# Local attention with global keys first in each 128-key set, overlapping value reads, one load of global parts a batch, and late expert weights

## The chip, the cores and the metric

The kernel runs on one core of a Trainium2 chip. The metric is the device time of one execution in microseconds (us), lower is better.

## What is computed

Three parts follow one another: local attention with global tokens, a mixture of four attention experts, and a channel mixing. Only the first and the weights of the second matter here (B = 4 batches, H = 8 heads, Sl = 512 local and Sg = 32 global tokens, head width 64, all float32):

```python
k_all = np.concatenate([k_g, k_l], axis=2)
v_all = np.concatenate([v_g, v_l], axis=2)
s_g = scale * np.matmul(q_g, k_all.transpose(0, 1, 3, 2))
out_g = np.matmul(sm(s_g), v_all)                      # sm: softmax
s_ll = scale * np.matmul(q_l, k_l.transpose(0, 1, 3, 2))
mask = np.abs(pos[:, None] - pos[None, :]) <= 32
s_ll = np.where(mask, s_ll, -1000000000.0)
s_lg = scale * np.matmul(q_l, k_g.transpose(0, 1, 3, 2))
a_l = sm(np.concatenate([s_lg, s_ll], axis=-1))
out_l = np.matmul(a_l, np.concatenate([v_g, v_l], axis=2))
```

The experts then use `moe_wq`, `moe_wk`, `moe_wv` (4 x 512 x 64 each), `moe_wo` (4 x 64 x 512) and `moe_w_gate` (512 x 4).

## The kernel before

**Tiling.** Each string of 32 local queries sees 32 global keys and at most 96 local ones, so its keys are a set of 128, and the keys' 128 rows are one contraction when the values are weighed. Four heads are a half of a batch (hf 0 and 1), two heads a pair. A *unit* u is half of the queries of a pair: 8 strings for each of 2 heads, 16 small matmuls of 32 rows of scores by 128 keys. A half has six steps: four units of local queries (v = 0 to 3), one of all global queries against all keys (v = 4), and one (v = 5) without scores of its own, in which the second part of the global result is turned and weighed. A batch has 12 steps (`UB`), and the four batches run through one software pipeline.

**Order.** Each engine has its own hand-written queue, and the engines meet at semaphores. At step i TensorE turns the probabilities of unit i-3 (`turn_probs`), perhaps keys, queries or global parts of what comes (tables `K_AT`, `Q_AT`, `G_AT`), turns back the result of unit i-6 (`turn_back`, tile `ps_X`), weighs values with unit i-4 (`weigh`, `ps_O`) and forms the scores of unit i (`scores`, `ps_S`). VectorE adds the mask and takes maxima (`maxima`), ScalarE takes exponentials and evicts (`exps`, `keep_probs`, `keep_out`). The global parts of the next batch's first half are turned at step 9; the first weighing of a half is at its steps 4 or 10.

**Keys.** The keys of a pair lie in `KS` as one string of 22 blocks of 32, in which a copy of the global keys stands every 128 columns, so each window of 128 columns holds the 32 global keys at some place (`window`). VectorE writes the local blocks (L592, L594), GpSimd the copies of the global ones (`keys_global`, L330).

**Values.** `VW` holds 14 windows of 128 rows in the same orders. `load_v` (L256) loads windows 0 to 4 and one quarter of window 9 in 11 transfers, and `copy_v` (L267) makes the others from them within SBUF by 6 more, which wait for all 11. `load_v` of batch b may start for a half when that half of batch b-1 has been weighed to its end (the semaphore `weighed`); for the second half this is step 3 of the following batch.

**The queue of SP.** All of these transfers are issued by SP, in order: for each batch queries, keys and global parts of both halves (`load_qk`), then loads and copies of values of the first half, then of the second. In batch 0 the 15 transfers of expert weights (L284 to L293) follow.

**Splitting of weights.** Each weight is split into a high part (ScalarE, L572) and a low one (GpSimd, L337), in 16 pieces at steps 6 to 11 of batch 0. The first split waits for all 15 transfers. The first use of the weights is behind the last batch, in `expert_projection`.

## Time and profile before

| what | value |
|---|---|
| median of 3 runs | 652.73 us (652.26 to 654.95) |
| the profiled execution | 655.85 us |
| span in the profile | 654.1 us |
| mean granted TensorE clock | 0.955 |
| busy: TensorE matmul, VectorE, ScalarE, GpSimd | 578.7, 321.4, 276.8, 96.3 us |
| attention stage | 0 to 186 us |
| its transfers | 36.2 MB in 75409 packets over the whole span, most of them of 256 bytes |

The waits show, for each engine, who made it idle; the timeline gives each group of instructions with its start; the windows give the busy time of each engine, the granted clock and the rate of the DMA engines for a stretch. A matmul in float32 leaves two records in the trace (x32 for 16 matmuls); a transpose leaves one. A row of the timeline gives start, duration of the whole group, engine, line, operation, and in brackets how long the engine had been idle and for whom.

### The profile page before, as it was taken

How to read it: one execution, taken by the hardware profiler on the slowest of the kernel's cores; microseconds unless marked ns; L12 is line 12 of the kernel's file. 1: busy time of each engine (PE TensorE's matmuls, PEld its weight loads, DVE VectorE, ACT ScalarE, POOL GpSimd, SP SyncE). 2: the span in 40 equal slices, each digit the busy share in tenths (PEclk: the TensorE clock that was granted, in tenths of full speed). 3: DMA queues.
4: the chain of work that ended last, by engine and by line, in shares of the span. 5: the costliest groups of instructions: out<-in, count | busy, mean ns of one | idle time of the engine just before them, and what ended most of it. 6: DMA issues, size and time to landing. Idle time of an engine off the chain costs nothing. (4 is left out here: it accounts for less than half of the span.)

```text
span 654.1 us, 16023 instructions
## 1 busy us (share of the span) xinstructions
PE 578.7 (88%) x6100; PEld 478.2 (73%) x6100; DVE 321.4 (49%) x807; ACT 276.8 (42%) x733; POOL 96.3 (15%) x189
## 2 busy tenths in 40 slices
PE   5718976896898899989989979799999999999998
PEld 3516654674685598779759749688989899898986
DVE  5424756575625435634653684754435344343412
ACT  3409756585645534533544453534133141322301
POOL 2006100010036412221232331300000000000000
PEclk9976989798999699989999998999999999999999
DMA  6697576766022100000000000400000000000000
GB/s 150 153 214 159 116 166 159 172 153 156 3 67 80 33 2 2 2 1 0 0 1 17 2 1 2 130 33 1 32 16 16 32 0 32 0 32 16 17 33 16
DMA packets 75409, 36.23 MB, mean 55 GB/s; under 512 B 68320, under 2 KB 68320, under 8 KB 75360
## 3 DMA queue, kind: packets, MB, share of 16 engines
q1 hardware_dynamic: 75360, 35.56, 22.0%
q8 instruction: 33, 0.54, 0.4%
q14 instruction: 16, 0.13, 0.1%
HBM read 21.77 MB, written 4.46 MB: 40 GB/s over the span
## 5 line engine op out<-in xcount | busy, mean ns | idle before, releaser
L44 PE MATMUL ps_H<-XH,w_kL 128*128 128x256 f32 (+1 forms) x288 | 81.5, 283 | 1.2 <-ACT square L1514 1.2
L1514 ACT ACTIVATE square<-ps_H 128x512 f32<-128x512 f32 (+1 forms) x36 | 20.5, 573 | 143.7 <-PE ps_H L46 141.6
L46 PE MATMUL ps_H<-XH,w_kH 128*128 128x256 f32 (+1 forms) x288 | 81.0, 281 | 0.0
L45 PE MATMUL ps_H<-XL,w_kH 128*128 128x256 f32 (+1 forms) x288 | 81.0, 281 | 0.0
L44 PEld LDWEIGHTS ps_H<-XH,w_kL 128*128 128x128 f32 x288 | 54.8, 190 | 2.1 <-ACT square L1514 1.4
L44 PE MATMUL ps_V<-w_vH,HL 128*128 128x512 f32 x136 | 53.8, 396 | 2.1 <-DVE HL L1566 2.1
L45 PEld LDWEIGHTS ps_H<-XL,w_kH 128*128 128x128 f32 x288 | 54.9, 190 | 0.4
L46 PEld LDWEIGHTS ps_H<-XH,w_kH 128*128 128x128 f32 x288 | 54.8, 190 | 0.0
L45 PE MATMUL ps_V<-w_vL,HH 128*128 128x512 f32 x136 | 53.7, 395 | 0.0
L46 PE MATMUL ps_V<-w_vH,HH 128*128 128x512 f32 x136 | 53.5, 394 | 0.0
L1582 DVE TENSOR_TENSOR square<-square 128x512 f32<-128x512 f32 (+1 forms) x36 | 24.4, 680 | 45.3 <-ACT square L1514 45.3
L1067 ACT ACTIVATE probs_m<-ps_H,nmax_m 128x128 f32<-128x128 f32 (+3 forms) x64 | 33.2, 523 | 31.0 <-DVE nmax_m L1221 30.9
L1599 DVE TENSOR_TENSOR gate<-ps_V,gate 128x512 f32<-128x512 f32 x17 | 11.8, 692 | 64.5 <-PE ps_V L46 64.5
L530 ACT ACTIVATE probs<-probs,nmax 128x128 f32<-128x128 f32 x128 | 40.7, 392 | 4.9 <-DVE nmax L623 4.9
L619 DVE TENSOR_TENSOR probs<-ps_S,mask 128x512 f32<-128x512 f32 x32 | 22.1, 691 | 40.9 <-PE ps_S L410 40.8
L538 ACT ACTIVATE PTs<-ps_P 128x512 f32<-128x512 f32 (+1 forms) x48 | 26.8, 559 | 34.5 <-PE ps_P L426 34.2
L1342 POOL TENSOR_SCALAR probs_m<-probs_m,rinv_m,coef 128x128 f32<-128x128 f32 (+3 forms) x64 | 39.2, 622 | 0.0
L449 PE MATMUL ps_O<-VW,PTs 128*32 128x65 f32 x1024 | 22.7, 233 | 15.8 <-DMA VW<-VW 14.9
L462 PE MATMUL ps_X<-ident,xn 128*128 128x128 f32 x72 | 15.8, 294 | 22.8 <-ACT xT L553 19.0
L449 PEld LDWEIGHTS ps_O<-VW,PTs 128*32 128x32 f32 x1024 | 17.5, 116 | 22.2 <-issue 20.7
L1221 DVE TENSOR_REDUCE nmax_m<-ps_H 128x1 f32<-128x128 f32 (+3 forms) x64 | 28.4, 484 | 10.9 <-PE ps_H L921 10.7
L44 PEld LDWEIGHTS ps_V<-w_vH,HL 128*128 128x128 f32 x136 | 25.9, 190 | 8.2 <-DVE HL L1566 2.6
(238 smaller groups left out, 1435.9 us busy)
## 6 DMA issues: line engine op xcount, KB each, us to landing
out_dram<-gate SPq DMA_DIRECT2D x17, 256.0 KB, 2.0
QKn<-in_k_l_dram SPq DMA_DIRECT2D x32, 128.0 KB, 2.6
QKn<-in_q_l_dram SPq DMA_DIRECT2D x32, 128.0 KB, 2.8
VW<-in_v_l_dram SPq DMA_DIRECT2D x40, 96.0 KB, 2.1
VW<-VW SPq DMA_DIRECT2D x24, 130.0 KB, 3.7
VW<-VW SPq DMA_DIRECT2D x8, 325.0 KB, 3.6
VW<-VW SPq DMA_DIRECT2D x8, 260.0 KB, 3.9
raw_b<-in_moe_w_k_dram SPq DMA_DIRECT2D x8, 256.0 KB, 2.8
```

The source lines that it names most:

```text
L44: nc.tensor.matmul(out, al, bh, start=(starts and k == 0), stop=False)
L45: nc.tensor.matmul(out, ah, bl, start=False, stop=False)
L46: last = nc.tensor.matmul(out, ah, bh, start=False, stop=(ends and k == n - 1))
L449: last = nc.tensor.matmul(out[SG * k:SG * k + SG, at:at + VD], PTs[:, u % 2, 2 * r + n, SG * k:SG * k + SG], VW[:, hf, w, 2 * (pair % 2) + ...
L530: last = nc.scalar.activation(pr, pr, ACT.Exp, bias=nmax[:, place(u), at:at + 1])
L538: nc.scalar.activation(PTs[:, u % 2, 0:n, :].rearrange("p j q -> p (j q)"), ps_P[:, u % 2, 0:P * n], ACT.Copy).then_inc(pt_kept, 1)
L619: nc.vector.tensor_tensor(pr, ps_S[:, :, 0:2 * P].rearrange("p r (n k) -> p r n k", n=2), mask[:, 2 * t:2 * t + 2, :, :].rearrange("p n a ...
L1067: nc.scalar.activation(probs[:, slot, r, 0:n], ps_S[:, r, 0:n], ACT.Exp, bias=nmax[:, slot, r:r + 1], accum_out=den[:, slot, r:r + 1]).the ...
L1221: nc.vector.tensor_reduce(nmax[:, slot, r:r + 1], ps_S[:, r, 0:n], AX.X, ALU.max, negate=True).then_inc(maxed, 1)
L1342: last = nc.gpsimd.tensor_scalar(pr, pr, rinv[:, slot, r:r + 1], coef[:, i, 2 * ep + r:2 * ep + r + 1], ALU.mult, ALU.mult)
L1514: nc.scalar.activation(square[:, g % 2, 0:2 * n], ps_H[:, g % 2, 0:2 * n], ACT.Relu).then_inc(relued, 1)
L1582: nc.vector.tensor_tensor(square[:, g % 2, 0:2 * n], square[:, g % 2, 0:2 * n], square[:, g % 2, 0:2 * n], ALU.mult).then_inc(squared, 1)
```

## The change

- The keys lie in `KS` as they come, 512 columns, evicted by one copy. The global keys stay in `GT`. Each set of 128 keys is now 32 global ones first, then 96 local ones, and its scores come from two matmuls: 96 columns from `KS`, 32 from `GT`. GpSimd's copies and the semaphore `kg_kept` go. The masks are the same in all strings but the first and the last.
- The values' window w is the 96 local rows from 32w on; all 14 are read from memory by one transfer per head (rows are read up to three times). The global rows are loaded once into window 0 and copied to the other 13 by one transfer.
- Global queries and keys come by two transfers a batch instead of four, behind the queries and keys of the first half.
- The expert weights come by 5 transfers instead of 15, issued behind the values of batch 1, and are split in 17 pieces at steps 2 to 10 of batch 3.
- A first exponential on ScalarE stands ahead of the first eviction.

```diff
@@ attention_phase @@
     def window(s):
-        c, kind = divmod(min(max(s, 1), 14) - 1, 3)
-        return 4 * c + (0, 2, 3)[kind], (0, 5, 10)[kind] + c
+        return min(max(s, 1), NW) - 1
...
-        SPLIT_FROM = 6
+        SPLIT_FROM = 2
...
         def split_at(b, i):
-            if isinstance(b, int) and b == 0 and i >= SPLIT_FROM:
+            if isinstance(b, int) and b == B - 1 and SPLIT_FROM <= i < UB:
...
+                def load_g(b):
+                    if b:
+                        sp.wait_ge(g_turned, 2 * b)
+                    for kind, glo in enumerate((qg_h, kg_h)):
+                        sp.dma_start(Gn[:, kind, :, :], glo[H * b:H * b + H, :, :].rearrange("h p d -> p h d")).then_inc(g_loaded, 16)
...
                 def load_v(b, hf):
-                    for c in range(5):
-                        sp.dma_start(VW[0:SG, hf, c, :, 0:DH], vg_h[h, :, :].rearrange("h p d -> p h d")).then_inc(v_loaded[hf], 16)
-                        sp.dma_start(VW[SG:P, hf, c, :, 0:DH],
-                                     vl_h[h, 96 * c:96 * c + 96, :].rearrange("h p d -> p h d")).then_inc(v_loaded[hf], 16)
-                    sp.dma_start(VW[96:P, hf, 9, :, 0:DH],
-                                 vl_h[h, SL - SG:SL, :].rearrange("h p d -> p h d")).then_inc(v_loaded[hf], 16)
+                    sp.dma_start(VW[0:SG, hf, 0, :, 0:DH], vg_h[h:h + 4, :, :].rearrange("h p d -> p h d")).then_inc(vg_loaded[hf], 16)
+                    for n in range(4):
+                        v = vl_h[h + n, 0:P - SG, :]
+                        sp.dma_start(VW[SG:P, hf, :, n, 0:DH],
+                                     bass.AP(v.tensor, v.offset, [[DH, P - SG], [SG * DH, NW], [1, DH]])).then_inc(v_loaded[hf], 16)
-                def copy_v(b, hf):
+                def copy_vg(b, hf):
                     sp.wait_ge(pool_set, POOL_SET)
-                    sp.wait_ge(v_loaded[hf], 16 * V_LOADS * (b + 1))
...
+                    sp.wait_ge(vg_loaded[hf], 16 * (b + 1))
+                    sp.dma_start(VW[0:SG, hf, 1:NW, :, :].rearrange("p w h d -> p w (h d)"),
+                                 VW[0:SG, hf, 0, :, :].rearrange("p h d -> p (h d)").unsqueeze(1)
+                                 .to_broadcast([SG, NW - 1, 4 * VD])).then_inc(vg_copied[hf], 16)
...
-                with sp.Fori(1, B) as b:
+                for b in range(1, B):
                     load_qk(b, 0)
+                    load_g(b)
                     load_qk(b, 1)
                     load_v(b, 0)
-                    copy_v(b, 0)
+                    copy_vg(b, 0)
                     load_v(b, 1)
-                    copy_v(b, 1)
+                    copy_vg(b, 1)
+                    if b == 1:
...
@@ scores @@
                     for n in range(2):
-                        for k in range(4):
...
-                                last = nc.tensor.matmul(ps_S[SG * k:SG * k + SG, r, P * n:P * n + P],
-                                                        QT[rows, pair % 2, SG * s:SG * s + SG], KS[rows, pair, at:at + P],
-                                                        start=True, stop=True)
+                        for local in (True, False):
+                            for k in range(4):
...
+                                    if local:
+                                        nc.tensor.matmul(out[:, SG:P], q, KS[rows, pair, at:at + P - SG], start=True, stop=True)
+                                    else:
+                                        last = nc.tensor.matmul(out[:, 0:SG], q, GT[rows, hf, pair % 2, :], start=True, stop=True)
...
@@ ScalarE, ahead of its first eviction @@
+                act.wait_ge(dve_set, 1)
+                nc.scalar.activation(nmax_g[:, 0:1], zerob[:, 0:1], ACT.Exp)
@@ keep_keys @@
-                    nc.vector.tensor_copy(KS[:, pair, 0:5 * P].rearrange("p (c k) -> p c k", k=P)[:, :, SG:P],
-                                          ps_T[:, 0:480].rearrange("p (c k) -> p c k", c=5))
-                    nc.vector.tensor_copy(KS[:, pair, 5 * P + SG:STRING], ps_T[:, 480:SL]).then_inc(k_kept, 1)
+                    nc.vector.tensor_copy(KS[:, pair, :], ps_T[:, :]).then_inc(k_kept, 1)
```

On TensorE, in batch 0 about its steps 6 and 7, the rows before are these (a name left of the arrow is the tile written, right of it the tiles read; sizes are partitions by columns):

```order
L449 MATMUL ps_O<-VW,PTs 32x65 x16
L410 MATMUL ps_S<-KS,QT 32x128 x16
L426 MATMUL ps_P<-ident,probs_g 128x128 x4
L376 MATMUL ps_T<-ident,QKn 128x128 x4
L462 MATMUL ps_X<-ident,xn 128x128 x2
```

and now:

```order
L438 MATMUL ps_O<-VW,PTs 32x65 x16
L398 MATMUL ps_S<-KS,QT 32x96 x8
L400 MATMUL ps_S<-GT,QT 32x32 x8
L398 MATMUL ps_S<-KS,QT 32x96 x8
L400 MATMUL ps_S<-GT,QT 32x32 x8
L414 MATMUL ps_P<-ident,probs_g 128x128 x4
L361 MATMUL ps_T<-ident,QKn 128x128 x4
L451 MATMUL ps_X<-ident,xn 128x128 x2
```

The 16 score matmuls of a unit have become 32, in four groups of 8; the rest stands where it stood.

On SP, before, the end of batch 0 with the second half's copies and the expert weights (the loop over batches 1 to 3 begins behind them):

```order
L264 DMA VW<-in_v_l_dram 32x4x64
L273 DMA VW<-VW 64x1300
L273 DMA VW<-VW 32x1300
L273 DMA VW<-VW 32x1040 x3
L273 DMA VW<-VW 64x1040
L284 DMA raw_qk<-in_moe_wq_dram 128x4x64 x4
L284 DMA raw_qk<-in_moe_wk_dram 128x4x64 x4
L287 DMA raw_v<-in_moe_wv_dram 128x4x64 x4
L289 DMA raw_v<-in_moe_w_gate_dram 128x4x4
L292 DMA raw_o<-in_moe_wo_dram 128x512 x2
```

and now, from the values of the second half of batch 1 to the global parts of batch 2:

```order
L264 DMA VW<-in_v_g_dram 32x4x64
L268 DMA VW<-in_v_l_dram 96x14x64 x4
L275 DMA VW<-VW 32x13x260
L296 DMA raw_qkv<-in_moe_wq_dram 128x16x64
L296 DMA raw_qkv<-in_moe_wk_dram 128x16x64
L296 DMA raw_qkv<-in_moe_wv_dram 128x16x64
L298 DMA raw_g<-in_moe_w_gate_dram 128x4x4
L299 DMA raw_o<-in_moe_wo_dram 128x2x512
L256 DMA QKn<-in_k_l_dram 128x4x64 x2
L256 DMA QKn<-in_q_l_dram 128x4x64 x2
L256 DMA QKn<-in_k_l_dram 128x4x64 x2
L256 DMA QKn<-in_q_l_dram 128x4x64 x2
```

The weights have moved a batch back, and the two transfers of `Gn` for batch 2 (L247) come right behind this piece.

## Rows read from the trace of the kernel before

**Rows 1.** Waits to 190 us: who waited for whom, us in total, times, longest.

```profile
ACT WQH L572 <- DMA raw_o<-in_moe_wo_dram: 15.4, 1, 15.4
PE ps_O L449 <- DMA VW<-VW: 14.9, 3, 5.4
...
PE ps_T L353 <- DMA Gn<-in_k_g_dram: 6.5, 2, 3.3
```

**Rows 2.** Timeline of TensorE: the first global-query matmuls of the eight halves.

```profile
26.62 1.87 PE L398 MATMUL ps_S<-KS,GQ 128*64 128x480 f32 x4
...
60.24 1.03 PE L398 MATMUL ps_S<-KS,GQ 128*64 128x480 f32 x4
...
75.75 1.03 PE L398 MATMUL ps_S<-KS,GQ 128*64 128x480 f32 x4
...
95.69 1.03 PE L398 MATMUL ps_S<-KS,GQ 128*64 128x480 f32 x4
...
116.64 1.87 PE L398 MATMUL ps_S<-KS,GQ 128*64 128x480 f32 x4
...
133.35 1.03 PE L398 MATMUL ps_S<-KS,GQ 128*64 128x480 f32 x4
...
153.33 1.87 PE L398 MATMUL ps_S<-KS,GQ 128*64 128x480 f32 x4
...
169.07 1.03 PE L398 MATMUL ps_S<-KS,GQ 128*64 128x480 f32 x4
```

**Rows 3.** Timeline of TensorE and SP's queue around the waits in batches 0 and 1.

```profile
51.23 0.66 PE L462 MATMUL ps_X<-ident,xn 128*128 128x128 f32 x2 [15.45 <-ACT xT L553]
...
69.71 0.41 PE L462 MATMUL ps_X<-ident,xn 128*128 128x128 f32 x2 [0.56 <-ACT xT L553]
...
72.91 0.43 PE L440 MATMUL ps_O<-VW,PTs 128*32 128x65 f32 x16
...
82.22 4.63 SPq L273 DMA_DIRECT2D VW<-VW  x6
87.66 0.32 SPq L247 DMA_DIRECT2D Gn<-in_q_g_dram  x1
...
90.27 0.19 PE L353 MATMUL ps_T<-zerob,identb 128*128 128x32 bf16 x1 [3.24 <-DMA Gn<-in_k_g_dram]
```

**Rows 4.** Timeline rows of small matmuls, and their own rows (ns min/median/max).

```profile
15.04 1.11 PE L410 MATMUL ps_S<-KS,QT 64*32 64x128 f32 x32 [0.85 <-DVE probs L619]
...
83.73 0.67 PE L410 MATMUL ps_S<-KS,QT 64*32 64x128 f32 x32
...
274.62 0.66 PE L954 MATMUL ps_Mm<-PTs_m,VS 128*64 128x32 f32 x16 [0.50 <-DVE PTs_m L1152]
...
L410 PE MATMUL ps_S<-KS,QT x1024: 269/269/420, 11.0 to 167.4; 64*32 64x128 f32 x171
...
L954 PE MATMUL ps_Mm<-PTs_m,VS x128: 214/223/315, 219.7 to 383.4; 128*64 128x32 f32 x128
```

**Rows 5.** Timeline of the start: ScalarE's table load, TensorE's first weighing.

```profile
4.14 1.28 ACT L503 ACT_TABLE_LOAD   x1 [4.14 <-PE ps_T L357]
...
25.59 1.10 PE L449 MATMUL ps_O<-VW,PTs 128*32 128x65 f32 x32 [4.76 <-DMA VW<-VW]
```

**Rows 6.** Windows: us, busy of PE, PEld, DVE, ACT, POOL; PEclk, DMA share, GB/s.

```profile
31.00:36.00 5.00, 4.78 (x147) 3.56 (x145) 4.15 (x12) 1.27 (x4) 0.00 (x0) 1.00 0.77 184
...
42.00:46.00 4.00, 0.00 (x0) 0.00 (x0) 0.00 (x0) 0.00 (x0) 0.00 (x0) 0.50 1.09 215
...
101.00:108.00 7.00, 6.33 (x200) 4.80 (x188) 5.08 (x14) 4.84 (x17) 0.00 (x0) 1.00 0.61 138
...
125.00:130.00 5.00, 4.37 (x144) 3.14 (x143) 4.00 (x11) 4.33 (x13) 0.00 (x0) 1.00 0.87 195
```

**Rows 7.** ScalarE's splits in the timeline, and a window of batch 3 (columns as above).

```profile
47.66 1.03 ACT L572 ACTIVATE WQH<-raw_qk 128x256 fp32r<-128x256 f32 x3 [15.39 <-DMA raw_o<-in_moe_wo_dram]
...
160.00:166.00 6.00, 5.30 (x170) 3.74 (x153) 5.37 (x13) 4.92 (x15) 0.00 (x0) 1.00 0.30 69
```

More of the change, by code:

```diff
@@ L276, in _ @@
+                load_g(0)
                 load_qk(0, 0)
@@ L337, in split_weights @@
                     nc.gpsimd.tensor_tensor(lo, src, hi, ALU.subtract).then_inc(w_split, 1)
-                def step(b, i):
-                    turn_at(b, i, K_AT, keys_global)
-                    for n in split_at(b, i):
-                        split_weights(n)
-                turn_at(0, -1, K_AT, keys_global)
-                run(pool, step, 0)
+                for n in range(len(pieces)):
+                    split_weights(n)
             @block.tensor
```

140 lines of the change are left out of this document (58 added, 82 removed).

## The prediction

> **What bounds the kernel now.** I read first the page, then the waits of the first 190 us, then the timeline of TensorE, last the DMA share by stage. TensorE is the busiest engine, but the change touches only the attention stage, the first 186 us; the code behind it is the same, so all terms lie in front. There the waits [rows 1] name three losses: 15.4 us in one piece, in which ScalarE waits for the last expert weight and holds up all that is queued behind it, TensorE's transpose at 51.23 among it [rows 3]; 14.9 us in three pieces in which the first weighing of a batch waits for the copied value windows; and 6.5 us for the global queries and keys (3.24 of it at 90.27).
>
> As a ruler I take the first global-query matmul (L398) of each half batch [rows 2]: 26.62, 60.24, 75.75, 95.69, 116.64, 133.35, 153.33, 169.07. The eight stand six steps apart. The one clean distance is 60.24 to 75.75, **15.5 us**. Seven of these would be 109 us; the rows show 142. What is over is the waits and the slow clock behind them: 51.23 to 60.24 took 9.0 us at a granted clock of 0.50 (the level of 1.2 GHz), while the same piece at full clock, 69.71 to 75.75, took 6.0 [rows 2, 3, 6]. So a long wait costs its length and about 3 us more, a wait of 5 us about 1.3 more (116.64 to 133.35 is 16.7).
>
> What feeds those waits is the SP queue. It works in order, 54 transfers a batch, and the copies of values can only be issued once the loads have landed: from the weighing that frees a half's values (ends 73.3) the values alone hold the queue until 86.9, and the next batch's loads start at 87.66 [rows 3]. From batch 2 to batch 3 the ruler shows 36.7 us against 31 for two clean halves.
>
> **The change part by part.**
>
> *Scores, more matmuls (cost).* Each of the 32 score groups goes from 16 matmuls to 32 (96 and 32 columns in place of 128). The trace shows two records for each such matmul, so 64 for 32. Two prices are possible. The group of 32 takes 0.67 us with a last record of 0.269: (0.67 - 0.269)/31 = 12.9 ns from one to the next [rows 4]. If the streamed columns set this, the total of columns stays and the cost is about nil. If the load of 32 stationary columns sets it, 32 more records cost 32 x 12.9 = 0.41 us. The nearest row with few streamed columns is L954: 32 of them behind 64 stationary ones, (0.66 - 0.214)/15 = 29.7 ns apart [rows 4]. By streamed columns it should be quicker than L410; it is twice as slow, and has twice the stationary columns. So I take **0.41 us per group**, with 0.03 and 0.60 (a whole group again) as ends. Global queries: 480+64 columns become 512+32, nothing. Per half four groups, 1.64 us. Of this one group fills the gap of half a us in which TensorE now waits for ScalarE (0.56 at 69.71) [rows 3], and a clean half becomes 15.5 + 1.64 - 0.4 = **16.8 us**.
>
> The Trainium skill, TensorEngine Tiling (Array Packing), section Performance Considerations, says against this that a matmul costs some 60 cycles however few columns it has. On eight tiles side by side 32 more records would then cost 32 x 60 / 8 cycles, 0.1 us by an estimate from that page, and the sum would be some 6 us better.
>
> *Values by overlapping reads.* Per half 17 transfers become 6. The bytes hardly move: 0.69 MB loaded and 1.16 MB copied before; 1.41 MB loaded and 0.43 MB copied now. But the copy needs only the small global load, so no landing stands in the queue, and the 4.63 us in which SP issues six copies [rows 3] become one issue. The DMA engines become the limit. Their rate when nothing holds them is 215 GB/s, at a share over 1; 184 at 0.77 with copies; 195 at 0.87; 138 at 0.61 where SP's small issues limit [rows 6]. I take 212 GB/s for all, and 195 and 224 as ends. Per half: values 8.7 us, queries and keys (1.05 MB) 4.9 us, together 13.6, less than 16.8. So the waits for values in front of 116.64 and 153.33, 5 us each, go.
>
> On this the Trainium skill, DMA: Bandwidth & Descriptors, section Specifications, has a rule: below 512 bytes a transfer does not reach line rate. Here 256-byte rows ran at 195 GB/s for a share of 0.87 and mostly 4 to 5 KB rows at 184 for 0.77, 224 against 239 per full share; were 256 bytes to run at half of the copies' rate, the sum would turn to a loss (third rival).
>
> *Start (A).* The table load (1.28 us) leaves the path [rows 5]; larger global loads give some back, -0.9. Four score groups at the low clock cost 4 x 0.68 (0.41 x 1.11/0.67), less the 0.85 us gap at 15.04 [rows 4]. TensorE came to the first weighing at 25.59 - 4.76 = 20.8 [rows 5], now 20.8 - 0.9 + 1.9 = 21.8. The values need 4.07 MB through the DMA engines: 0.8 + 0.4 + 19.2 + 2.6 = 23.0. L398 about 1.1 later, 24.1: **-2.5**.
>
> *Weights late.* In batch 0 the 15.4 us wait and its slow clock go. But the same 2.1 MB now stand in the SP queue behind the values of batch 1's second half and **ahead of batch 2's queries, keys and global parts**. SP may issue those values only once the last weighing of batch 0 is done (step 3 of batch 1). In the trace: weighing ends at 73.3, global load issued at 87.66, in use at 90.27, where TensorE had waited 3.24 [rows 3]. Now, counted from that weighing: values 1.84 MB, weights 2.11, queries and keys 1.05, at 212 GB/s 23.6 us, and 2.7 for issue, transfer and landing of the global parts (87.66 to 90.27): 26.3. TensorE wants them at step 9, 87.0 - 73.3 = 13.7 us after the weighing before, now some 15.0 (four score groups more, less the gap). **Wait of about 11.4 us in batch 1.** Without weights (batch 2) it is 13.6 + 2.7 = 16.3 against 15.0: 1.3. In batch 0: 6.96 MB from the start, 0.8 + 0.4 + 32.8 + 2.6 = 36.6, against L398 + 12.1 = 36.2 for TensorE: 0.4.
>
> *One load of global parts.* Same bytes, 2 issues fewer; but it now stands behind the queries and keys instead of ahead of them, 4.9 us later. Counted above; it is what makes the two small waits.
>
> *ScalarE in batch 3.* 17 splits of some 0.31 us (1.03 us for three) move from batch 0, where they ran beside stalled work, to steps 2 to 10 of batch 3. ScalarE is busy 4.92 of 6.00 us there [rows 7], 2.1 of a step of 2.6. Two splits add 0.6 and the longer step, 2.8, leaves 0.7: it just fits, so each late piece now reaches TensorE. From 0 to 4 us (the 4.9 that the splits take, less what is free); I take 1.0. *VectorE, GpSimd:* the key eviction is one copy instead of two, the 16 fills by GpSimd go, the masks are 14 small writes instead of 32 and end before the first sum: nothing on the path, as TensorE does not wait for them.
>
> **The sum**, half by half (now minus before): A -2.5; B 33.6 to 16.8 + 0.4 + 0.7 of slow clock (half of 1.3), -15.7; C 15.5 to 16.8, +1.3; D: the weighing that frees the values ends 2.4 + 0.4 before L398, the wait 26.3 after it (23.5 after L398), then 4.3 + 0.4 + 2.8 of slow clock to the next L398, 31.0 for 19.9, +11.1; E 16.8 + 0.7 for 20.95, -3.4; F 16.8 + 1.3 for 16.7, +1.4; G 16.8 for 19.98, -3.2; H 16.8 + 1.0 for 15.7, +2.1. Together **-8.9 us**. The profiled execution took 655.85 us (span 654.1), 3 us above the median; I put the difference on the median: 652.73 - 8.9 = **643.8 us**.
>
> **The rivals.**
> 1. *Score matmuls cost nothing* (columns bound them). C, E, G, H lose 1.2 each, B and F some 0.8, since there the DMA engines set the time: -15.3, 637.4 us. Against it L954. The Trainium skill leans this way with the 60 cycles of its page TensorEngine Tiling (Array Packing), section Performance Considerations.
> 2. *The DMA engines give 195 GB/s*, as in the mixed stage. B +2.9, D +2.0, F +1.2, and waits of 2.6 us at step 9 of batches 0 and 2 now bring the low clock, as the 3.24 us one did, 1.3 each: about 652.7 us, no change. The gain is given back as waits for global parts.
> 3. *The value reads are slow* (**slower than before**). They are 5376 packets of 256 bytes per half for 2688, in steps of 8 KB in memory. Each extra us per half lands on A, B, D and F and brings slow clock of 3 to 4 us in all: the sum turns when a half's reads take some 1.5 to 2 us more than 6.5, below 165 GB/s. At 140 GB/s they take 9.8: +13 and +4, 661 us. For it: nothing in the rows, all loads are of 256 bytes already. Against: 215 GB/s for expert weights, most of them in 256-byte rows.
> 4. *ScalarE sets batch 3*: its end of 4 us instead of 1, and one spell of slow clock, 1.3: 648.1 us.
>
> **How the numbers follow.** Forecast 0.45 (640 to 648), rival 1 0.16, rival 2 0.15, rival 3 0.13, rival 4 0.11. The range takes in 1, 2 and 4 and leaves 3 out: 635 to 656 us. A measurement of this kernel tells about 0.5% from no change, 3.3 us. Faster than 649.5: forecast, rival 1 and most of 4, 0.70; within: rival 2 and the rest, 0.16; slower 0.14.
>
> **What would show it.** The score group's two rows together: 1.08 us or 0.70. TensorE's wait for Gn at step 9 of batch 1, about 11 us, under 2 in batches 0 and 2; none for VW after the first. Clean halves of 16.8 us; the DMA rate over 200 GB/s while values load; the last L398 near 160. A wait for VW in later batches, or a wait for Gn over 3 us in batch 2, would show the value reads slower than I took them. If the prediction is wrong by much, the likely step is the wait behind the weights, the largest term that is only worked out.

## The result and the profile after

The changed kernel takes **661.32 us** (median of 9 runs, 658.63 to 663.21) against 652.73 (9 runs): ratio 1.0125, interval 1.0103 to 1.0148. It is slower by 8.6 us where 8.9 us less were forecast, and the time lies outside the range of 635 to 656. The profiled run has a span of 661.0 us. Attention ends at 193.0 us instead of 186, so nearly all of the difference stands where the forecast put all of its terms. Executions more than 1.5% above the fastest of their kernel are left out of every median and ratio in this document (one of four of a_wide_gap_gfirst, three of eleven of a_gap_gfirst and three of ten of a_unroll, among the experiments below).

TensorE's rows after the change: six of the eight ruler matmuls (L382 now, to be laid beside [rows 2]) and every stop of over 1 us between 5 and 150 us.

```profile
24.92 1.09 PE L438 MATMUL ps_O<-VW,PTs 128*32 128x65 f32 x32 [4.16 <-DMA VW<-VW]
25.95 1.98 PE L382 MATMUL ps_S<-KS,GQ 128*64 128x512 f32 x4
...
42.09 0.19 PE L338 MATMUL ps_T<-zerob,identb 128*128 128x32 bf16 x1 [3.05 <-DMA Gn<-in_k_g_dram]
...
47.53 1.08 PE L382 MATMUL ps_S<-KS,GQ 128*64 128x512 f32 x4
...
64.67 1.08 PE L382 MATMUL ps_S<-KS,GQ 128*64 128x512 f32 x4
...
77.73 1.08 PE L429 MATMUL ps_O<-VW,PTs 128*32 128x65 f32 x29 [2.39 <-issue]
...
89.41 0.20 PE L338 MATMUL ps_T<-zerob,identb 128*128 128x32 bf16 x1 [9.37 <-DMA Gn<-in_k_g_dram]
...
95.33 1.08 PE L382 MATMUL ps_S<-KS,GQ 128*64 128x512 f32 x4
...
104.63 1.11 PE L414 MATMUL ps_P<-ident,probs 128*128 128x128 f32 x4 [6.41 <-issue]
...
119.49 1.08 PE L382 MATMUL ps_S<-KS,GQ 128*64 128x512 f32 x4
...
135.51 0.21 PE L338 MATMUL ps_T<-zerob,identb 128*128 128x32 bf16 x1 [2.62 <-DMA Gn<-in_k_g_dram]
...
142.20 1.08 PE L382 MATMUL ps_S<-KS,GQ 128*64 128x512 f32 x4
```

The last two L382 stand at 159.38 and 176.06. Piece by piece (A is the time up to the first of them, B to H are the distances from one to the next):

| | A | B | C | D | E | F | G | H | last L382 |
|---|---|---|---|---|---|---|---|---|---|
| forecast | 24.1 | 17.9 | 16.8 | 31.0 | 17.5 | 18.1 | 16.8 | 17.8 | 160.0 |
| measured | 25.95 | 21.6 | 17.1 | 30.7 | 24.2 | 22.7 | 17.2 | 16.7 | 176.06 |
| miss | +1.9 | +3.7 | +0.3 | -0.3 | +6.7 | +4.6 | +0.4 | -1.1 | +16.1 |

The clean halves (C, G) and the piece with the big wait behind the weights (D) came out near the forecast. Three pieces carry most of the miss. B and F end in waits for `Gn`, as the forecast had them, but of 3.05 and 2.62 us for 0.4 and 1.3. And in E stands something that it didn't have at all: at 104.63 TensorE had been idle for 6.41 us, "issue", that is, for nothing that the profile shows. No such row is in the kernel before. L414 there is the first work of a pass of TensorE's loop over batches 1 and 2: the stop is at the jump back to the loop's start.

Two views tell more. First the page's DMA queues (packets, MB, share of the 16 engines). Of the kernel before:

```profile
q1 hardware_dynamic: 75360, 35.56, 22.0%
q8 instruction: 33, 0.54, 0.4%
...
HBM read 21.77 MB, written 4.46 MB: 40 GB/s over the span
```

Of the changed kernel:

```profile
q1 hardware_dynamic: 97472, 35.47, 25.8%
q8 instruction: 49, 0.80, 0.6%
...
HBM read 27.54 MB, written 4.46 MB: 48 GB/s over the span
```

The data queue moves the same bytes in 29% more packets. And q8, an instruction queue with packets of 16 KB, has 49 packets instead of 33; the runs below show that it follows the length of TensorE's code. Between 100 and 140 us, the loop's second pass, the kernel before fetches none and the changed one nine. The DMA view of these 40 us of the changed kernel:

```profile
DMA packets 16641, 4.95 MB, mean 124 GB/s; under 512 B 15800, under 2 KB 16632, under 8 KB 16632
...
q8 instruction: 9, 0.15, 1.9%
```

Second, windows of the changed kernel (columns as in [rows 6]): batch 0's loads, two places where value reads run nearly alone, and one where weights, queries and keys run.

```profile
20.00:40.00 20.00, 13.92 (x396) 10.47 (x394) 9.64 (x26) 8.85 (x24) 0.00 (x0) 1.00 1.07 184
61.00:67.00 6.00, 5.31 (x145) 3.86 (x138) 3.77 (x10) 4.21 (x13) 0.00 (x0) 1.00 0.79 148
...
116.00:122.00 6.00, 5.31 (x145) 3.96 (x145) 3.77 (x10) 4.21 (x13) 0.00 (x0) 1.00 0.74 151
...
80.00:89.40 9.40, 0.04 (x3) 0.00 (x0) 1.38 (x2) 0.00 (x0) 0.00 (x0) 0.50 1.06 219
```

The forecast went by 212 GB/s. For weights, queries and keys that holds (219). In batch 0, with value reads in the mix and a share over 1, so with engines that have nothing in reserve, there were 184. SP needed 4.88 and 5.92 us there to issue four value loads (5.64 at 61.64, where nothing else was being loaded), and 2.51 instead of 1.00 for two key loads right behind the first four. SP's queue in the timeline (start, time for the issue):

```profile
1.74 1.00 SPq L256 DMA_DIRECT2D QKn<-in_k_l_dram  x2
...
6.63 4.88 SPq L268 DMA_DIRECT2D VW<-in_v_l_dram  x4
11.55 2.51 SPq L256 DMA_DIRECT2D QKn<-in_k_l_dram  x2
...
21.48 5.92 SPq L268 DMA_DIRECT2D VW<-in_v_l_dram  x4
27.50 1.60 SPq L275 DMA_DIRECT2D VW<-VW  x1
...
37.99 0.50 SPq L247 DMA_DIRECT2D Gn<-in_q_g_dram  x1
```

So `Gn` of batch 1 is issued at 38 us and in use at 42.09, where the forecast had 36.6.

### The profile page after: what moved, and what is told of

Read it like the earlier page. It is cut to its first block and busy times, and to the rows that moved or that the text cites. A ratio compares the mean times of both kernels' runs of the same rounds, so it can differ in the third digit from the quotient of the medians.

```text
span 661.0 us, 17698 instructions
## 1 busy us (share of the span) xinstructions
PE 589.3 (89%) x7124; PEld 493.2 (75%) x7124; DVE 320.4 (48%) x773; ACT 277.3 (42%) x735; POOL 87.1 (13%) x173
## 5 line engine op out<-in xcount | busy, mean ns | idle before, releaser
L952 PEld LDWEIGHTS ps_Ym<-PTs_m,VS 128*64 128x64 f32 x320 | 18.4, 144 | 19.3 <-DVE PTs_m L1137 11.6
L398 PE MATMUL ps_S<-KS,QT 64*32 64x96 f32 x1024 | 30.3, 281 | 1.9 <-issue 1.1
L414 PE MATMUL ps_P<-ident,probs 128*128 128x128 f32 x128 | 25.0, 327 | 6.4 <-issue 6.4
```

Of the source, the lines that this page charges most:

```text
L398: nc.tensor.matmul(out[:, SG:P], q, KS[rows, pair, at:at + P - SG], start=True, stop=True)
L414: last = nc.tensor.transpose(ps_P[:, u % 2, P * n:P * n + P], src, ident[:])
```

## The experiments

My first theory was that both the waits for `Gn` and the stop at the jump come from the full DMA queue (instructions stuck behind deep value reads). The rival was that the stop belongs to the score split, which doubles the number of TensorE's score matmuls. All times are medians; the kernel before gave 651.9 to 653.1 us in the five sets of runs, and each ratio is to the kernel before of the same set.

| run | us | ratio to before | q8 packets | TensorE idle for issue to 200 us |
|---|---|---|---|---|
| kernel before | 652.7 | 1 | 33 | 0.9 |
| the change | 661.3 | 1.0125 (1.0103 to 1.0148) | 49 | 13.0 |
| a_gap | 655.7 | 1.0050 (1.0020 to 1.0081) | 49 | 14.9 |
| a_gfirst | 652.4 | 1.0015 (0.9984 to 1.0047) | 49 | 14.6 |
| a_gap_gfirst | 646.3 | 0.9886 (0.9852 to 0.9920) | 49 | 17.1 |
| a_vlate | 663.8 | 1.0214 (1.0136 to 1.0291) | 49 | 12.9 |
| b_split | 665.4 | 1.0205 (1.0166 to 1.0245) | 49 | 9.4 |
| a_one | 650.8 | 0.9953 (0.9919 to 0.9987) | 33 | 0.8 |
| a_one_gap_gfirst | 635.4 | 0.9753 (0.9704 to 0.9801) | 33 | 1.7 |
| a_wide | 669.6 | 1.0255 (1.0192 to 1.0317) | 44 | 9.3 |
| a_wide_gap_gfirst | 646.9 | 0.9898 (0.9831 to 0.9965) | 44 | 10.7 |
| a_unroll | 658.2 | 1.0045 (1.0005 to 1.0085) | 47 | 17.8 |
| b_unroll | 656.4 | 1.0057 (1.0027 to 1.0088) | 39 | 3.5 |
| b_pad | 698.3, one run | | 43 | 5.3 and the added waits |
| a_copy | 661.7 | 1.0115 (1.0057 to 1.0172) | 49 | 8.4 |
| a_copy_gap_gfirst | 646.4 | 0.9899 (0.9858 to 0.9939) | 49 | 11.9 |
| b_direct | 666.5 | 1.0210 (1.0167 to 1.0252) | 33 | 0.9 |
| b_rest | 644.2 | 0.9845 (0.9803 to 0.9887) | 33 | 0.9 |
| b_rest_split | 655.4 | 1.0062 (1.0033 to 1.0091) | 49 | 11.4 |
| b_rest3 | 642.4 | 0.9846 (0.9803 to 0.9889) | 33 | 0.9 |

The last column sums the rows of the waits that put TensorE's idle time down to issue. It is no price by itself: part of such a stop only shortens a wait that would come behind it, so a_unroll has more of it than the change and is still faster. Names with a_ start from the change, with b_ from the kernel before.

### Where the weights and the global parts stand in the queue

a_gap moves the weights' five transfers from behind batch 1 to between the two value halves of batch 2, a place where SP waits anyway:

```diff
                     copy_vg(b, 0)
+                    if b == 2:
+                        for kind, w in enumerate((moe_wq, moe_wk, moe_wv)):
...
                     load_v(b, 1)
                     copy_vg(b, 1)
-                    if b == 1:
-                        for kind, w in enumerate((moe_wq, moe_wk, moe_wv)):
...
```

> The changed kernel with the five weight transfers issued between the two halves of batch 2's values (where SP waits 15 us for the weighing) instead of behind batch 1. Theory 1 (the place of the weights costs the wait): the wait for Gn at step 9 of batch 1 falls from 9.4 us to the 2.6 us that batch 2 shows, its slow clock goes, 8 us less: 653 us, and 647 if the 6.4 us in which TensorE waits for nothing shown at the start of batch 2 goes too. Theory 2 (TensorE's own instructions come late behind deep data transfers): that piece stays, at 3 to 6 us, since the values of batch 2 are still in the queue when the loop jumps back. Rival: the weights are on no path, then it stays at 661.

a_gfirst only swaps two calls:

```diff
-                    load_qk(b, 0)
                     load_g(b)
+                    load_qk(b, 0)
                     load_qk(b, 1)
```

> The changed kernel with the load of global parts ahead of the queries and keys of the first half. If the place behind 1 MB of queries and keys makes the waits for Gn, those of batches 0 and 2 (3.0 and 2.6 us) go to nil and that of batch 1 falls by 4 to 5 us: some 10 us less with the slow clock, 651 us. If the waits are only passed on to the keys that are turned one step later, 2 to 4 us less.

a_gap gained 5.6 us of the 8 expected, a_gfirst 8.9 of some 10. With the global parts first, TensorE's waits for `Gn` in batches 0 and 2 are gone and only batch 1's stays, behind the weights. Its timeline in a_gfirst:

```profile
83.73 0.20 PE L338 MATMUL ps_T<-zerob,identb 128*128 128x32 bf16 x1 [7.20 <-DMA Gn<-in_k_g_dram]
...
97.81 1.11 PE L414 MATMUL ps_P<-ident,probs 128*128 128x128 f32 x4 [5.45 <-issue]
```

The stop at the jump is still there, at 97.81. Both moves together:

> The changed kernel, same computation, with the weights' transfers between the value halves of batch 2 and the global parts' transfers ahead of the queries and keys. The Gn waits (15 us in the change) go to under 1.5 us, the standstill at TensorE's jump (4 to 6.5 us) and the group's 0.23 us stay. If the two orders only share the wait of batch 1: 650 to 653 us, as the global parts alone; if each takes a wait of its own: 645 to 649 us. a_wide_gap_gfirst gave 649.3 us; if the wide matmul costs there what it cost in a_wide (8 us), this run is at 641 us.

646.3 us: 15.0 less than the change, the sum of the two (14.5). The moves don't share a gain. No wait for `Gn` after the first remains, and the kernel is 1.1% faster than before, with the stop at the jump at 5.59 us.

### What makes the stop at the jump

a_vlate holds back the value reads of batch 2's first half until the jump is over:

```diff
+                    if b == 2:
+                        sp.wait_ge(scored, 10 * b + 1)
                     load_v(b, 0)
```

> The changed kernel with one more wait on SP: the values of batch 2's first half are issued only when the first scores of batch 2 are done, so that no value load is in the queue when TensorE jumps back to the loop's start. Theory 2 (instructions come late behind deep data transfers): the 6.4 us piece at the jump goes; the values then come 1 to 4 us late at step 4; 656 to 661 us. Rival (it is another wait that the trace does not name): the piece stays and the values come later besides, 664 us or more.

663.8 us; the held values now make TensorE wait for `VW` too, 2.26 us at 122.50. TensorE still stands at the jump, as its timeline in a_vlate shows:

```profile
102.66 1.11 PE L416 MATMUL ps_P<-ident,probs 128*128 128x128 f32 x4 [3.92 <-issue]
```

And yet from 97 to 103 us the DMA engines now carried three packets, all of them instructions (two on q8, one on q14, the other instruction queue); the DMA view of these 6 us:

```profile
DMA packets 3, 0.04 MB, mean 7 GB/s; under 512 B 0, under 2 KB 0, under 8 KB 0
...
q8 instruction: 2, 0.03, 2.7%
```

So data in the queues doesn't make the stop; at most it adds to it (6.41 us in the change for 3.92 here, one trace each). My first theory fell here. b_split goes the other way, the kernel before with its score matmuls cut and nothing else:

```diff
+                        for lo, hi in ((SG, P), (0, SG)):
                             for k in range(4):
...
-                                last = nc.tensor.matmul(ps_S[SG * k:SG * k + SG, r, P * n:P * n + P],
-                                                        QT[rows, pair % 2, SG * s:SG * s + SG], KS[rows, pair, at:at + P],
+                                    last = nc.tensor.matmul(ps_S[SG * k:SG * k + SG, r, P * n + lo:P * n + hi],
+                                                            QT[rows, pair % 2, SG * s:SG * s + SG], KS[rows, pair, at + lo:at + hi],
```

> The kernel before with each score matmul cut in two (96 and 32 columns), in the order of the changed kernel, nothing else. My step had 0.41 us a group of scores and 1.3 us a clean half. The trace after shows groups of 0.83 to 0.95 us instead of 0.60. If that is the price, clean halves grow by 0.8 to 1.2 us, the SP-bound ones by nothing: 655 to 658 us. If the streamed columns set it: 653 us.

It took 665.4 us, 13.5 more than the kernel before and 7 above the expectation, which had priced the matmuls alone, with 49 packets of instructions and a stop of 5.01 us at the jump. It also gives the price of the split on the engine itself. A group of scores in the timeline of b_split starts at 71.36 and the next work at 72.18:

```profile
71.36 0.89 PE L411 MATMUL ps_S<-KS,QT 64*32 64x96 f32 x64
72.18 0.19 PE L353 MATMUL ps_T<-zerob,identb 128*128 128x32 bf16 x1
```

That is 0.82 us; in the kernel before such a group takes 0.60 (70.83 to 71.43). In the change, too, most groups at the full granted clock take 0.82 or 0.83, and six with stops inside take 1.38 to 1.74.

a_one is the reverse inside the change: one matmul of 128 local keys, without the global keys' scores.

```diff
-                                    if local:
-                                        nc.tensor.matmul(out[:, SG:P], q, KS[rows, pair, at:at + P - SG], start=True, stop=True)
-                                    else:
-                                        last = nc.tensor.matmul(out[:, 0:SG], q, GT[rows, hf, pair % 2, :], start=True, stop=True)
+                            at = min(SG * window(s), SL - P)
...
+                                last = nc.tensor.matmul(ps_S[SG * k:SG * k + SG, r, P * n:P * n + P],
+                                                        QT[rows, pair % 2, SG * s:SG * s + SG], KS[rows, pair, at:at + P],
+                                                        start=True, stop=True)
```

> The changed kernel with one 128-column score matmul per 32 queries again in place of the 96 + 32 columns: it reads 128 local keys of KS, and the scores of the global keys are left out, so the output is another; everything else (value reads, loads, queue order, early table load) is as in the change. If the split is the step that failed, both the 0.23 us that a group of 16 takes longer and the standstill of 4 to 6.4 us at the jump back to the loop's start go: the group is back at 0.60 us, TensorE's transposes at the jump wait for nothing, the instruction queue carries no packet in the loop's second pass, and the time falls by what the split cost the kernel before, 13.5 us: about 648 us. Rival: the loads do it (more packets, weights later), and the split only shows it: then the anchors move by no more than the matmuls themselves, 64 units x 2 groups x 0.23 us less what is hidden, and the time stays above 655 us with the standstill at the jump still there.

650.8 us, 10.5 less, with 33 packets, no stop and groups of 0.60 us. Is it the matmuls or the length of the loop? b_pad puts as many instructions into the loop as the split does (a float32 matmul leaves four records, two of weight loads and two of matmuls; 128 more matmuls a batch make 512), and no work in them:

```diff
+                    if i == 9 and not isinstance(b, int):
+                        for _ in range(512):
+                            pe.wait_ge(dve_set, 3)
```

> The kernel before with 512 semaphore waits that are already fulfilled put into TensorE's loop body ahead of the global parts' turn for the next batch: as many instructions as the score split adds to the body, with no work in them. They take TensorE's time at their own place, so the whole time says little; it is the jump that tells. If the size of the body is the cause, a standstill put down to issue of 4 us or more stands at the jump between batch 1 and 2 (none in the kernel before) and the instruction queue has 8 to 16 packets more than 33. If it is the matmuls, the jump has no standstill.

TensorE's stops in the timeline of b_pad:

```profile
113.82 0.20 PE L353 MATMUL ps_T<-zerob,identb 128*128 128x32 bf16 x1 [27.97 <-issue]
126.39 1.11 PE L426 MATMUL ps_P<-ident,probs 128*128 128x128 f32 x4 [3.91 <-issue]
```

The first row is the price of the waits themselves, 55 ns each. The second is the jump: 3.91 us, what a_vlate had (3.92), though here data was still moving during the first half of the stop; the page counts 43 packets. It is one execution, but the stop and the packets are read off its trace, not off its time. **The length of the loop body makes the stop.** The kernel before fits: its second pass fetches nothing. The longer body doesn't, so its second pass fetches anew, and at the jump nothing is there yet. The packets also tell the size, as an estimate: one more pass written out costs the kernel before 6 packets (b_unroll, below, 39 for 33), and with all four batches written out the split costs 8 more (a_unroll, 47 for 39), 2 a batch. So a body of some 6 packets stays and one of some 8 doesn't. By that b_pad has 33 + 2 + 8 = 43, as counted; b_split would have 33 + 6 + 8 = 47 against 49. The Trainium skill, Runtime: NRT & Kernel Launch, section Terms, describes each engine's instruction memory as 32 to 128 KiB, refilled in blocks of 16 KiB; the packets here are of that size (0.54 MB in 33).

Writing TensorE's loop out, and no other engine's, takes the jump away, in the change (a_unroll) and in the kernel before (b_unroll):

```diff
-            with eng.Fori(1, B - 1) as b:
+            for b in range(1, B - 1):
                 for i in range(UB):
                     step(b, i)
```

> The changed kernel with TensorE's loop over batches 1 and 2 written out: the same instructions with no jump, the other engines' loops as they are. Theory 1, the standstill is the refetch at the jump's target, and straight code is fetched ahead of its use: the standstill at the end of batch 1 goes, the time falls by 4 to 6.5 us to 655 to 657 us, the group stays 0.83 to 0.95 us. Theory 2, fetching itself is too slow while data is moving: the pieces put down to issue remain, spread over the second pass, and the time stays within 1.5 us of 661 us. Theory 3, the standstill is no fetch but a wait on a semaphore that the trace doesn't show: it stays where it is.

> The kernel before with TensorE's loop over batches 1 and 2 written out, nothing else: the instruction queue gets the packets of one more pass of the body (33 to about 40) and there is no jump. If fetching straight code is hidden behind the work, the time stays within 1.5 us of 652.5 us; if fetching is what costs (pieces put down to issue of 0.7 to 3.6 us, as in a_unroll), 656 to 662 us.

Neither expectation of a free fetch held. a_unroll is at 658.2 us, with a wide spread (650.6 to 660.0), 3 us under the change by the medians where 4 to 6.5 were expected (its ratio would put it at 656): the jump's stop became many smaller ones, the longest 3.63 us, together 17.8 us. b_unroll lost 3.6 us to the kernel before with six packets more. In the table the idle time for issue goes with the packets: 0.8 to 1.7 us at 33, 3.5 at 39, 5.3 at 43, 8.4 and more from 44 on. Here straight code is not hidden behind the work either, probably because a float32 matmul of 32 rows is over so soon (13 ns a record, [rows 4]); that cause was not tried apart.

### Fewer, wider matmuls

If the number of instructions costs, then four 32 x 32 matmuls with the same keys may be one: the global keys are the same for all queries.

```diff
-                                        last = nc.tensor.matmul(out[:, 0:SG], q, GT[rows, hf, pair % 2, :], start=True, stop=True)
+                        for r in range(2):
+                            rows, sq = slice(64 * r, 64 * r + 64), P * (2 * t + n)
+                            last = nc.tensor.matmul(ps_S[:, r, P * n:P * n + SG], QT[rows, pair % 2, sq:sq + P],
+                                                    GT[rows, hf, pair % 2, :], start=True, stop=True)
```

> The changed kernel, same computation, with the global keys' scores of 128 queries made by one matmul of 128 weight columns and 32 moving columns per half of the array, in place of four of 32 x 32: a group is 10 matmuls instead of 16 (before: 8). If the number of TensorE's instructions is what costs, nearly all comes back: group 0.62 to 0.72 us, standstill at the jump gone or under 2 us, time 649 to 653 us. If the number of the loop's instructions still is over what stays in the engine, the standstill stays (4 us or more) and only the group's length comes back: 655 to 659 us. If it is the narrow moving side (32 columns) that costs, the group stays above 0.8 us and the time above 657 us.

669.6 us, worse than the change by 8.3. In the timeline of a_wide a unit of scores starts at 71.71 and the next work at 73.04:

```profile
71.71 0.40 PE L394 MATMUL ps_S<-KS,QT 64*32 64x96 f32 x16
72.03 0.41 PE L399 MATMUL ps_S<-GT,QT 64*128 64x32 f32 x4
72.38 0.40 PE L394 MATMUL ps_S<-KS,QT 64*32 64x96 f32 x16
72.70 0.41 PE L399 MATMUL ps_S<-GT,QT 64*128 64x32 f32 x4
73.04 0.66 PE L414 MATMUL ps_P<-ident,probs_g 128*128 128x128 f32 x4
```

That is 1.33 us for 20 matmuls, where the change mostly has 0.82 for 32 and the kernel before 0.60 for 16. The small matmuls overlap: a record of L394 lasts at least 239 ns, and 16 of them fill 0.32 us. Two matmuls (four records) across the array's whole width take 0.35 us, more than those 16. The rows of the weight loads (ns min/median/max) for 128 stationary columns in a_wide, and for 32 in the change:

```profile
L399 PEld LDWEIGHTS ps_S<-GT,QT x256: 182/186/330, 10.3 to 182.4; 64*128 64x128 f32 x128
...
L400 PEld LDWEIGHTS ps_S<-GT,QT x1024: 102/107/175, 10.4 to 174.4; 64*32 64x32 f32 x171
```

Two such loads of 186 ns for each half of the array's rows come to 0.37 us, about what the wide part takes (an estimate). And with 44 packets the loop still doesn't fit. The third theory of the expectation has the numbers, but not the cause: the 32 moving columns the change has too. What is new is the 128 stationary ones; no run tried another width.

The wide matmul together with both moves in the queue:

> The changed kernel with the wide matmul for the global keys' scores, the weights' five transfers issued between the two value halves of batch 2 instead of behind batch 1, and the global parts' transfers issued ahead of the queries and keys. If the three causes add up (weights' place 5.6 us, global parts' place 8.9 us with 3 of them common to both, split some 8 to 10 us): 641 to 646 us, with all waits for Gn under 1 us. If the value reads then set the end (wait for the values' load ahead of the weighing of over 3 us in more than one batch): 647 to 652 us.

646.9 us (644.1 to 651.7, three executions), not to be told from the 646.3 of a_gap_gfirst. So the wide matmul costs less there than the 8.3 us here; where it hides was not followed up.

### The value reads

a_copy puts the values' old way into the change: 6 loads and 4 copies a half for the local rows.

```diff
-                        sp.dma_start(VW[SG:P, hf, :, n, 0:DH],
-                                     bass.AP(v.tensor, v.offset, [[DH, P - SG], [SG * DH, NW], [1, DH]])).then_inc(v_loaded[hf], 16)
+                    for c in range(5):
+                        sp.dma_start(VW[SG:P, hf, 3 * c, :, 0:DH],
+                                     vl_h[h:h + 4, 96 * c:96 * c + 96, :].rearrange("h p d -> p h d")).then_inc(v_loaded[hf], 16)
...
+                    sp.wait_ge(v_loaded[hf], 16 * V_LOADS * (b + 1))
+                    for to, n, w, count, at, src in ((32, 64, 1, 5, 64, 0), (96, 32, 1, 4, 32, 3), (32, 32, 2, 4, 96, 0), (64, 64, 2, 4, 32, 3)):
...
```

> The changed kernel, same computation, where only the local values come otherwise: 5 loads of 96 rows and one of 32 a half, and 4 copies inside the chip that fill the windows between, as in the kernel before but in the change's window order; the values' global part as in the change. Theory 1, the overlapping reads are slower than the forecast's 212 GB/s and push the queue back, so Gn's waits of batches 1 to 3 (9.4, 2.6, 3.1 us) shrink: time 654 to 658 us. Theory 2, the reads pay as forecast (waits for the copies return, about 4 us a piece ahead of the weighing): 664 to 670 us. Theory 3, the one makes up for the other: within 2 us of 661 us.

> a_gap_gfirst (646.3 us) with the values loaded and copied as in a_copy. It differs from b_rest (644.2 us) by the window order, and with it the split of the scores, alone. If the overlapping reads pay once the queue's order is mended: 649 to 655 us, with waits for VW of 4 us a half back. If they cost: 640 to 645 us. And if the split costs its 10 us here too, b_rest is that much below this one: 654 us.

661.7 against 661.3 and 646.4 against 646.3: **the overlapping reads bring or cost nothing that can be measured.** The third theory of a_copy held. They run at 148 to 151 GB/s when alone, slower than I took them, and save the landing between load and copy; that the one pays for the other is a reading, not a test. In the same stretch of batch 0, from 20 to 40 us, a_copy's engines give 187 GB/s at a share of 0.95, and `Gn` of batch 1 is in use at 41.98 us, for 184 and 42.09 in the change:

```profile
20.00:40.00 20.00, 13.38 (x395) 9.87 (x393) 9.45 (x26) 8.64 (x24) 0.00 (x0) 1.00 0.95 187
```

So 212 GB/s was too high for batch 0 with either way of getting the values. The `Gn` waits of batches 1 and 2 even grew, to 14.13 and 5.43 us, while the stops for issue shrank. a_copy_gap_gfirst was expected 10 us above b_rest (below), for the split; it is 2.2 above, and the next section comes back to that.

b_direct and b_rest start from the kernel before and keep its windows and its score matmuls. Both take over from the change the global parts once a batch (ahead of the queries and keys, as in a_gfirst), the weights in five transfers (in the gap of a_gap) with their split in batch 3, and the early table load. b_rest keeps the 11 loads and 6 copies of values; b_direct reads overlapping, and since the windows have their old order there, it needs 20 loads of local rows a half, one load and 3 copies of global ones.

```diff
+                    for to, n, w, count, at in ((SG, 96, 0, 5, 0), (0, 64, 5, 5, 32), (96, 32, 5, 5, 96), (0, 32, 10, 4, 64), (64, 64, 10, 4, 96)):
+                        for k in range(4):
+                            v = vl_h[h + k, at:at + n, :]
+                            sp.dma_start(VW[to:to + n, hf, w:w + count, k, 0:DH],
+                                         bass.AP(v.tensor, v.offset, [[DH, n], [96 * DH, count], [1, DH]])).then_inc(v_loaded[hf], 16)
```

> The kernel before with everything of the change but its score split: the windows of 128 keys stay as they are laid out before (global keys inside each string, 16 score matmuls a unit, TensorE's 1655 rows of work), but all 14 value windows are read straight from memory by overlapping reads (20 loads a half), the values' global part is loaded once and copied by 3 copies, global parts once a batch and ahead of the queries and keys, the weights in 5 transfers between the two value halves of batch 2, split in batch 3, the function table loaded early. Theory 1, the split was the step that failed and the rest brings what the forecast gave it: the instruction queue has 33 packets, no standstill at the jump, and the time is 640 to 645 us. Theory 2, the value reads at 148 to 151 GB/s eat the gain: waits for VW ahead of the weighing of 3 us and more in batches 1 to 3, time 648 to 653 us.

> As b_direct, but the values by the 11 loads and 6 copies inside the chip of the kernel before; so it tells what the overlapping reads are worth, all else equal. Theory 1 (reads pay): the waits for VW<-VW ahead of the weighing stay (15 us in three pieces before) and the time is 646 to 650 us, 4 to 7 us above b_direct. Theory 2 (reads cost, 185 GB/s against 224 for a full share, 5.8 MB more from memory): the time is at or below b_direct, 640 to 645 us.

b_rest gives 644.2 us, b_direct 666.5. b_rest's number is that of its second theory. SP needs 12.66 us for the 20 loads, where four with the same bytes took 4.88; SP's row in the timeline of b_direct:

```profile
6.63 12.66 SPq L271 DMA_DIRECT2D VW<-in_v_l_dram  x20
```

In b_direct TensorE waits for values in all four batches, for 20.1 us (14.0 in b_rest), and what stands behind them in the queue comes late too: 14.6 us of waits for `Gn` (9.9 in b_rest) and 7.0 for keys (none). The row of its waits for values:

```profile
PE ps_O L457 <- DMA VW<-VW: 20.1, 4, 6.4
```

My expectation of b_direct had looked at bytes and rates only; it missed by over 20 us, and its pessimistic theory by 13.5.

### Does the split cost the same everywhere?

b_rest_split is b_rest with the cut of b_split; a_one_gap_gfirst is a_gap_gfirst with the matmuls of a_one. b_rest3 moves b_rest's weights one batch further (`b == 3`, `SPLIT_FROM = 4`).

> b_rest (644.2 us) with each 128-column score matmul cut into 96 and 32 columns, as in b_split. If the split's price is its own (0.23 to 0.35 us a unit on 32 units, 7 to 11 us, and 4 to 5 us at the jump), it is there in every setting: 655 to 658 us. If most of it is the collision with transfers that come late anyway, it shrinks with the waits: 646 to 649 us, with the standstill of 4 us and more at the jump still there and the wait for Gn in batch 3 shorter by as much.

> a_gap_gfirst (646.3 us) with the score matmuls of a_one: 128 local keys in one matmul, the scores of the global keys left out, so another output. If the split costs 8 to 13 us here too: 634 to 638 us. If what it costs is mostly hidden behind loads: 641 to 646 us, with a longer wait for Gn or VW in its place.

> b_rest with the weights' five transfers between the value halves of batch 3 instead of batch 2 (their split into parts begins four units into batch 3 instead of two). If the weights' place makes the wait of 6.6 us for Gn in batch 3, it goes: 638 to 642 us. If the split of the weights then ends late and the first projection waits for it (w_split), 644 us and more.

The split's price by medians is 13.5 us (b_split), 10.5 (a_one), 11.2 (b_rest_split) and 10.9 (a_one_gap_gfirst). Each is good to some 3 us, so the four can't be told apart: the price is the split's own and hides nowhere. b_rest3 is at 642.4 us. Its wait for `Gn` in batch 3 is under 1 us, but the weights now land too late for their first split. ScalarE stands 9.57 us for the last of them, and TensorE behind it 5.12 us, the same chain as the 15.4 us wait of [rows 1]; the timelines of ScalarE and of TensorE in b_rest3:

```profile
144.50 1.03 ACT L575 ACTIVATE WQH<-raw_qkv 128x256 fp32r<-128x256 f32 x3 [9.57 <-DMA raw_o<-in_moe_wo_dram]
...
146.55 1.11 PE L371 MATMUL ps_T<-ident,QKn 128*128 128x128 f32 x4 [5.12 <-ACT QT L517]
```

It can't be told from b_rest (0.9846 and 0.9845). These two are the fastest complete kernels of the study, 1.5% ahead of the kernel before.

a_copy_gap_gfirst (646.4) and b_rest_split (655.4) have the same split, the same queue order and copied values. The 9.0 us between them are the change's plain layout: 12 transfers a half for values instead of 17 (the global rows loaded once and copied), one eviction of keys, no fills by GpSimd, fewer writes of masks. Which of these it is wasn't tried apart.

## Why the prediction was wrong

**What held, in part by luck.** Rival 1, matmuls for nothing, is refuted: an undisturbed score group grew from 0.60 us to 0.82. But that is +0.22 where the forecast had +0.41. The clean halves of 16.8 still came out at 17.1 and 17.2, since each holds groups with fetch stops that the forecast didn't have: the four of C took 0.82, 0.82, 0.83 and 1.54 us, 1.6 more than four of 0.60, as the forecast's 1.64. The wait behind the weights in batch 1, the term that I trusted least: 9.37 us and 2.39 us of issue ahead of it, for 11.4. D as a whole is within 0.3 us, but of two misses that cancel: from the issue of the values (61.29) to `Gn` in use (89.41) it took 28.1 us for 26.3, and from there to the next L382 5.9 for 7.5. The 15.4 us wait of ScalarE [rows 1] went, as did the waits for values of batches 1 to 3. H was 1.1 us better than feared, so rival 4 is refuted too.

**The step that failed in size: 212 GB/s for all transfers.** It came from a window in which expert weights were loaded ([rows 6], 215 at 1.09), and for weights, queries and keys it was right (219). With values in the mix the engines give 184 at a share of 1.07 and about 150 where value reads are alone. From this, `Gn` of batch 1 is in use at 42.09 instead of 36.6, and waits of 0.4 and 1.3 us became 3.05 and 2.62, each with slow clock behind it. With the values' later arrival in A that is most of the 10.2 us by which A, B and F missed; F also holds 1.2 us of stops for issue. This is rival 2's mechanism, and the rate fell below its 195. Rival 3 gave 661 us from value reads of 140 GB/s, close to both numbers, but it isn't what happened: with the old loads and copies (a_copy) the time is the same 661.7. What turned the slow rate into waits was the place of `load_g`. The prediction named it ("it is what makes the two small waits") and priced it at 1.7 us; a_gfirst measured 8.9. The rate alone was harmless where the order didn't put `Gn` last.

**The step that was missing: the size of TensorE's code.** The split was priced as time on the engine and nothing else. It also makes the loop body too long to stay: 6.41 us at the jump, most of E's 6.7, and smaller stops in every batch. The profile before had the signs, 33 instruction packets and none in the loop's second pass; I didn't read that row of the page. Rival 1 against the forecast put the split at 6.4 us in all, and it costs 10.5 inside the change. The matmuls themselves are the smaller part of it: 32 groups at 0.22 us, less the gap of 0.4 in each of the eight halves that the forecast let them fill, are about 4 us (an estimate), so some 6 are left for fetching instructions.

**The balance.** 661.3 less 10.5 for the split and 15.0 for the order would be 635.8; a_one_gap_gfirst, with both, has 635.4. The forecast was 643.8: with the misses of A, B and F it would have come to about 654 (643.8 + 10.2), and with E's to 661. This adds up measured pieces and is no test of its own.

## What to carry over

Before a loop's body is made longer, look at the instruction queue: if a later pass of the loop fetches nothing, the body fits, perhaps just, and more instructions, however cheap, may bring a stop at every jump and the fetch of each pass. Count matmuls on small tiles by what shares the array; merging them into one that takes the whole width can be slower. When transfers share one in-order queue, put the small ones that the next step needs first, and price the order with a pessimistic rate: here two moves of calls were worth 15 us, while the new way of reading the values brought nothing. And look at where a moved load is needed: b_rest3 only traded one wait for another.

## What was not expected of the hardware

- At the jump of a loop that doesn't fit, TensorE stood 3.9 us where the DMA engines carried only instructions (a_vlate), as long in b_pad, where they were idle for the second half of the stop, and 4.8 to 6.7 us with data moving all the while (a_copy, a_gap).
- A wait that is already fulfilled costs TensorE some 55 ns (27.97 us for 512, b_pad).
- A value read that steps through memory in 256-byte rows ran at 148 to 151 GB/s at a share of 0.74 to 0.79; per full share that is 187 to 204, against 224 for the loads of [rows 6].
- 20 loads took SP 12.66 us to issue where 4 loads with the same bytes took 4.88: some 0.5 us for each more.
